# A gated linear attention and two MLPs on one core: the first step of the recurrence loaded and ordered another way, and v issued by another queue

## The chip, the cores and the metric

One core of one Trainium2 chip runs the whole program. The metric is the device time of that core in microseconds. The kernel before takes 954.99 us, the median of three runs (954.11 to 955.01). The execution that the profile shows took 954.32 us, and its span, from the first to the last recorded instruction, is 952.2 us.

## What is computed

```python
f = 1.0 / (1.0 + np.exp(-f_logit))            # q, k, v, f: 4 batches, 8 heads, 768 tokens, 48 columns
for t in range(S):
    state = f[:, :, t, :, None] * state + np.einsum('bhd,bhe->bhde', k[:, :, t], v[:, :, t])
    y[:, :, t] = np.einsum('bhd,bhde->bhe', q[:, :, t], state)
x = y.transpose(0, 2, 1, 3).reshape(B * S, H * D)      # 3072 tokens, 384 columns
x = (sigmoid(x @ w_gate) * (x @ w_val)) @ w_out        # 384 -> 1536 -> 384
h = x @ w_in                                           # 384 -> 2048
out = (h * sigmoid(1.702 * h)) @ w_out2                # 2048 -> 384
```

## The kernel before

The recurrence is cut into 12 steps of 64 tokens. A step has four units, one for each pair of heads (UG = 4), and a unit holds the four batches side by side: 256 columns (W) on 2 x 48 partitions. Units are numbered through, so units 0 to 3 are the first step, 4 to 7 the second. For a unit ScalarE makes the gates (`forget`), VectorE makes two products of gates by scans (`begin_decay`, `end_decay`), GpSimd multiplies k and q by them (`decay_k`, `decay_q`), and TensorE works in visits. A visit turns k of one unit (`k_turned`, copied by `take_k`), makes its scores, which VectorE masks, and in the same visit or the next one makes the y and the new state of a unit whose scores are masked. ScalarE copies y out of PSUM (`take_y`), for later steps VectorE adds the part within the step (`add_y`), and DMAs of SyncE move y to its rows of x (`move_y`, two or three DMAs a unit, as the 48 rows of a head cross a slab of 128).

The MLPs run over groups of tokens: two groups of 256 (steps 0 and 1), then groups of 512. A group of the first MLP has twelve blocks of 128 hidden columns. Every product is made of three matmuls in the fp32r format (w_hi by x_hi, w_hi by x_lo, w_lo by x_hi), so a block is 9 matmuls for the gate, 9 for the value and 9 for the output of the block before. x and the weights are split for it into hi (ScalarE casts) and lo (VectorE subtracts): `x_first_part` and `x_second_part`, `w1_first_part` and `w1_second_part`. The weights of the first MLP come in twelve pieces of 1152 columns that pass through three slots in `stage` and one in `final`; they are loaded and split ahead of their blocks in group 0.

Before the first block TensorE makes eight visits, which bring step 0's y into x. Later visits lie between the value and the output of blocks named in `VISIT_AT`: five in group 0 (they make the y of step 1), eight in group 1 (the y of steps 2 and 3, which group 2 reads), eight in each later group. `FORGET_AT` and `PREPARE_AT` say in which block the gates and the decays of a unit are made. Each engine runs its list in order. In block q ScalarE makes the sigmoid, waits for VectorE's product, casts `act_hi`, and then does what else is due (`take_k`, `forget`, `take_end`, `take_y`, a piece of w1, at block 10 `x_first_part` of the next group). TensorE may start the gate of block q only when the sigmoid of block q - 1 is done (`sig_done`), and its value when VectorE's product of block q - 1 is done (`mul_done`). Where x of a new group is split, ScalarE waits in its list for every y that has to be there (`y_moved`), and its next sigmoid stands behind that.

SyncE's list in a block with a visit is `load_f` of a coming unit, `load_kq`, `load_v`, `move_y` of the unit just made, in an order that depends on the block. All are DMAs of SyncE's one queue; each costs that queue its issue time. ScalarE's queue issues w1 from piece 1 on and, for the first step, f and v. At the start SyncE loads k and q of units 0 to 3 one unit after another, w1 piece 0, then moves y; ScalarE loads f and v unit by unit in between its work. TensorE's `keep_warm(n)` makes n products that nobody reads. Before the first block TensorE waits for all moves of y.

## Time and profile before

| | |
|---|---|
| median of 3 runs | 954.99 us |
| the profiled execution | 954.32 us |
| its span | 952.2 us |
| TensorE busy | 931.2 us, 98% |
| VectorE, ScalarE, GpSimd busy | 45%, 35%, 11% |
| first matmul of the first MLP | 28.57 us |

The page gives the totals; the timelines give what happened when. In a timeline an instruction has its start, its duration, its line of the kernel, what it writes and reads, and in brackets how long its engine had been idle before it and who ended that. SPq and ACTq are DMA issues in the lists of SyncE and ScalarE. A matmul's duration overlaps its neighbour's, so the pace of TensorE is read from the distance of two starts. The granted clock of TensorE is 1.00 at 2.4 GHz and 0.50 at 1.2 GHz.

### The profile page before, as it was taken

Reading aid. Unit: us, or ns where it says so; the run is one execution under the profiler, and the core shown is the slowest. Engines: PE = TensorE matmul, PEld = TensorE weight load, DVE = VectorE, ACT = ScalarE, POOL = GpSimd, SP = SyncE. Lnnn points to the kernel's source line nnn. Section 1 sums busy time; section 2 is a strip of 40 time slices with the busy share of each in tenths; the row PEclk is TensorE's granted clock in tenths of the full one; section 3 lists DMA queues with packets and bytes.
Section 4 is the critical chain, followed back from the end, with each engine's and each line's share of the span. In section 5 each row is a group of like instructions: output and inputs, shape, how many; then the busy total and the mean of one; then the engine's idle time right before and its main releaser. Section 6 shows DMA issues by size and latency. Waiting matters only on the chain.

```text
span 952.2 us, 17778 instructions
## 1 busy us (share of the span) xinstructions
PE 931.2 (98%) x7147; PEld 779.8 (82%) x7147; DVE 433.1 (45%) x789; ACT 335.9 (35%) x753; POOL 107.0 (11%) x126
## 2 busy tenths in 40 slices
PE   7899979999999999999999999999999999999997
PEld 5899968888888888888888888888888888888886
DVE  5697645437445544644333234343443443443433
ACT  3564433334333333333324333332232332232332
POOL 4112211102111111211004420000000000000000
PEclk6899989999999999999999999999999999999999
DMA  5863322222321321130223330010010200200000
GB/s 142 220 164 70 78 66 62 57 48 51 73 50 40 78 64 43 34 88 15 63 67 100 100 84 0 1 67 1 16 52 0 67 1 1 67 0 1 34 1 35
DMA packets 108374, 52.34 MB, mean 55 GB/s; under 512 B 95488, under 2 KB 100096, under 8 KB 108288
## 3 DMA queue, kind: packets, MB, share of 16 engines
q1 hardware_dynamic: 103312, 43.67, 18.2%
q10 hardware_dynamic: 4976, 7.49, 2.6%
q8 instruction: 58, 0.95, 0.4%
q14 instruction: 28, 0.23, 0.1%
HBM read 36.96 MB, written 9.44 MB: 49 GB/s over the span
## 4 chain that ended last, share of the span: by engine, by line
PE 92%; SPq 2%; DMA 2%; ACTq 1%; ACT 1%; DVE 1%; issue 1%; DVEq 0%
PE up_ps L1080 17%; PE up_ps L1082 17%; PE up_ps L1081 17%; PE out_ps L1080 13%; PE out_ps L1081 12%; PE out_ps L1082 12%; DMA f_raw<-f_t 2%; PE att_ps L1046 2%; PE att_ps L1064 1%; PE att_ps L1073 1%; PE att_ps L1055 1%; PE turn_ps L1025 1%; SPq L413 1%; SPq L406 1%; SPq L382 1%
## 5 line engine op out<-in xcount | busy, mean ns | idle before, releaser
L1080 PE MATMUL up_ps<-x_hi,w_hi 128*128 128x512 f32 (+1 forms) x792 | 294.9, 372 | 9.5 <-ACT act_f L710 9.5
L1082 PE MATMUL up_ps<-x_hi,w_lo 128*128 128x512 f32 (+1 forms) x792 | 294.4, 372 | 0.0
L1081 PE MATMUL up_ps<-x_lo,w_hi 128*128 128x512 f32 (+1 forms) x792 | 294.3, 372 | 0.0
L1080 PE MATMUL out_ps<-act_hi,w_hi 128*128 128x512 f32 (+1 forms) x540 | 207.8, 385 | 0.7 <-DVE act_lo L941 0.7
L1081 PE MATMUL out_ps<-act_lo,w_hi 128*128 128x512 f32 (+1 forms) x540 | 203.0, 376 | 0.0
L1082 PE MATMUL out_ps<-act_hi,w_lo 128*128 128x512 f32 (+1 forms) x540 | 202.6, 375 | 0.0
L716 ACT CAST act_hi<-act_f 128x512 fp32r<-128x512 f32 (+1 forms) x180 | 106.6, 592 | 234.4 <-DVE act_f L927 162.1
L1080 PEld LDWEIGHTS up_ps<-x_hi,w_hi 128*128 128x128 f32 x792 | 150.4, 190 | 35.3 <-ACT act_f L710 7.0
L1082 PEld LDWEIGHTS up_ps<-x_hi,w_lo 128*128 128x128 f32 x792 | 150.3, 190 | 25.6
L1081 PEld LDWEIGHTS up_ps<-x_lo,w_hi 128*128 128x128 f32 x792 | 150.4, 190 | 25.5
L941 DVE TENSOR_TENSOR act_lo<-act_f,act_hi 128x512 fp32r<-128x512 f32 (+1 forms) x180 | 117.7, 654 | 78.7 <-ACT act_hi L716 78.7
L927 DVE TENSOR_TENSOR act_f<-act_f,up_ps 128x512 f32<-128x512 f32 (+1 forms) x84 | 51.2, 610 | 210.9 <-PE up_ps L1082 205.1
L930 DVE TENSOR_TENSOR act_f<-act_f,up_ps 128x512 f32<-128x512 f32 x96 | 66.0, 687 | 173.4 <-ACT act_f L712 173.4
L712 ACT ACTIVATE act_f<-up_ps 128x512 f32<-128x512 f32 x96 | 57.4, 598 | 193.0 <-PE up_ps L1082 193.0
L1080 PEld LDWEIGHTS out_ps<-act_hi,w_hi 128*128 128x128 f32 x540 | 101.8, 189 | 22.0 <-DVE act_lo L941 1.2
L1082 PEld LDWEIGHTS out_ps<-act_hi,w_lo 128*128 128x128 f32 x540 | 101.9, 189 | 18.6
L1081 PEld LDWEIGHTS out_ps<-act_lo,w_hi 128*128 128x128 f32 x540 | 101.9, 189 | 17.1
L710 ACT ACTIVATE act_f<-up_ps 128x512 f32<-128x512 f32 (+1 forms) x84 | 45.0, 536 | 128.9 <-PE up_ps L1082 128.5
L543 POOL TENSOR_TENSOR k_dec<-k_raw,after_prod 128x256 f32<-128x256 f32 x48 | 41.7, 868 | 313.0 <-DVE after_prod L801 240.6
L642 ACT COPY y_t<-att_ps 48x128 f32<-48x128 f32 x176 | 45.7, 260 | 16.2 <-DVE state L839 14.7
L811 DVE TENSOR_TENSOR_SCAN to_prod<-gate,starts 128x264 f32<-128x264 f32 x44 | 40.2, 913 | 0.0
L533 POOL TENSOR_TENSOR q_dec<-q_raw,to_prod 128x256 f32<-128x256 f32 x48 | 33.0, 687 | 54.8 <-issue 42.9
(74 smaller groups left out, 516.5 us busy)
## 6 DMA issues: line engine op xcount, KB each, us to landing
stage<-w SPq DMA_DIRECT2D x16, 384.0 KB, 3.3
k_raw<-k_t SPq DMA_DIRECT2D x96, 48.0 KB, 2.1
q_raw<-q_t SPq DMA_DIRECT2D x96, 48.0 KB, 2.1
stage<-w ACTq DMA_DIRECT2D x8, 576.0 KB, 4.4
x_dram<-final SPq DMA_DIRECT2D x36, 128.0 KB, 2.4
x_raw<-x_dram SPq DMA_DIRECT2D x6, 768.0 KB, 4.7
out_t<-final SPq DMA_DIRECT2D x18, 256.0 KB, 2.3
v_raw<-v_n SPq DMA_DIRECT2D x88, 48.0 KB, 2.3
```

Source lines behind the costliest of these rows:

```text
L543: pool.tensor_tensor(by_chunk(k_dec[:, u.s, :]), by_chunk(k_raw[:, u.s, :]), chunks(after_prod, u.s)[:, :, 2:], ALU.mult).then_inc(k_dec_d ...
L642: last = act.copy(y[rows[i], :, r, :], banks(v)[rows[r], i, STATE_COL:STATE_COL + BLOCKS * C].rearrange("p (c t) -> p c t", c=BLOCKS))
L710: act.activation(act_f[:, b.t, 0:b.n], up_ps[:, 0, 0:b.n], ACT.Sigmoid).then_inc(sig_done, 1)
L712: act.activation(act_f[:, b.t, 0:b.n], up_ps[:, b.j % 2, 0:b.n], ACT.Sigmoid, scale=1.702).then_inc(sig_done, 1)
L716: act.copy(act_hi[:, b.t, 0:b.n], act_f[:, b.t, 0:b.n]).then_inc(act_hi_done, 1)
L811: dve.tensor_tensor_scan(to_prod[:, u.s, :], gate_of(n), starts[:, u.s, :], 1.0, ALU.mult, ALU.max).then_inc(scan_done, 1)
L927: dve.tensor_tensor(act_f[:, b.t, 0:b.n], act_f[:, b.t, 0:b.n], up_ps[:, 1, 0:b.n], ALU.mult).then_inc(mul_done, 1)
L930: dve.tensor_tensor(act_f[:, b.t, 0:b.n], act_f[:, b.t, 0:b.n], up_ps[:, b.j % 2, 0:b.n], ALU.mult).then_inc(mul_done, 1)
L941: dve.tensor_tensor(act_lo[:, b.t, 0:b.n], act_f[:, b.t, 0:b.n], act_hi[:, b.t, 0:b.n].bitcast(F32), ALU.subtract).then_inc(act_split, 1)
L1080: pe.matmul(dst, w_hi[:, at:at + P], m_hi, start=first, stop=False)
L1081: pe.matmul(dst, w_hi[:, at:at + P], m_lo, start=False, stop=False)
L1082: return pe.matmul(dst, w_lo[:, at:at + P], m_hi, start=False, stop=last)
```

## The change

- The first step's f, k and q come in one pair of DMAs each for all four units (f of unit 0 also by itself, ahead), and v in four DMAs, all issued by SyncE. They land in space that is free so early: f in `act_f`, k in the slot of w1 piece 2, q in the slot of piece 3. So piece 2 is loaded by SyncE after the four `decay_k` and three `move_y`, and piece 3 by ScalarE after the four `decay_q`. The slots of later units are cleared by GpSimd instead.
- The visits of the first step are split into parts and ordered anew: scores of units 0 and 1, y of 0, scores of 2, y of 1, scores of 3, y of 2 and 3; only then the states of 0 to 3, with the turns of k of units 2 and 3. There are twelve visits instead of eight, with the same products in sum. They use more PSUM banks, and the two decay products of units 2 and 3 have places of their own.
- Of each unit's y the first head (rows 0 to 47) is copied from PSUM straight into x, by ScalarE for units 0 and 1 and by VectorE for 2 and 3 (`put_y`); the second head is moved by DMA as before, so there are five moves in step 0 instead of ten.
- The states of step 0 are copied by ScalarE (`take_state`), the casts of the first three pieces of w1 are made by GpSimd, and `take_end` goes from ScalarE to GpSimd for all units.
- Unit 4's gates are still made ahead of the first block, but its decays are now made in block 0 of group 0, its visit lies in block 1 instead of 0, and the other visits of group 0 in blocks 3, 4, 6, 8 instead of 2, 4, 6, 8.
- From group 1 on `load_v` is issued by ScalarE, right after `take_y`, instead of by SyncE ahead of `move_y`.
- TensorE makes five unread products behind each of the first four `after_done`, and other numbers of them later.

```diff
-    VISITS = []
-    for n in range(UG):
-        VISITS += [(n, None), (None, n)]
+
+    VISITS = [(0, 0, None, None), (1, 1, None, None), (None, None, None, 0), (None, 2, None, None), (None, None, None, 1),
+              (None, 3, None, None), (None, None, None, 2), (None, None, None, 3),
+              (None, None, 0, None), (2, None, 1, None), (3, None, 2, None), (None, None, 3, None)]
     BEFORE_MLP = len(VISITS)
...
+    VISITS += [(UG, UG, None, None)] + [(n, n, n - 1, n - 1) for n in range(UG + 1, UNITS)] + [(None, None, UNITS - 1, UNITS - 1)]
...
-        for j in (0, 2, 4, 6, 8) if g == 0 else (0, 1, 3, 4, 5, 7, 8, 9):
+        for j in (1, 3, 4, 6, 8) if g == 0 else (0, 1, 3, 4, 5, 7, 8, 9):
...
-            FORGET_AT.update({(g, j): n + 6 for n, j in enumerate((0, 2, 4, 6, 8, 10))})
-            PREPARE_AT.update({(g, j): n + 5 for n, j in enumerate((0, 2, 4, 6, 8, 10))})
+            FORGET_AT.update({(g, j): n + 5 for n, j in enumerate((0, 1, 3, 5, 7, 9, 11))})
+            PREPARE_AT.update({(g, j): n + 4 for n, j in enumerate((0, 1, 2, 4, 6, 8, 10))})
...
+                sp.wait_ge(gaps_set, 1)
+                for i in range(PAIR):
+                    sp.dma_start(by_batch(f_raw[rows[i], 0, :]), f_steps[0, i, :, :, 0:C]).then_inc(f_loaded[0], 16)
+                sp.wait_ge(gaps_set, 2)
+                for i in range(PAIR):
+                    sp.dma_start(all_units(f_first[rows[i], :]), f_units[i, :, :, 0:C]).then_inc(first_f_loaded, 16)
                 sp.wait_ge(gaps_set, 3)
-                load_k(0)
+                for i in range(PAIR):
+                    sp.dma_start(all_units(k_first[rows[i], :]), k_units[i, :, :, 0:C]).then_inc(first_k_loaded, 16)
                 sp.wait_ge(q_gaps_set, 1)
-                load_q(0)
-                for n in range(1, UG):
-                    load_kq(n)
+                for i in range(PAIR):
+                    sp.dma_start(all_units(q_first[rows[i], :]), q_units[i, :, :, 0:C]).then_inc(first_q_loaded, 16)
+                for r in range(SIDES):
+                    for c in range(BLOCKS):
+                        sp.dma_start(v_raw[halves[r], 0:UG, c, :], v_units[r, c, 0:C, :, 0, :]).then_inc(first_v_loaded, 16)
                 sp.dma_start(w1_staged(0), w1[:, 0:PIECE1]).then_inc(w1_loaded[0], 16)
+                load_f(4)
+                load_kq(4)
                 move_y(0)
-                load_k(4)
                 move_y(1)
-                load_q(4)
-                move_y(2, slice(2, 3))
-                move_y(3, slice(1, 2))
-                load_v(4)
+                move_y(2)
+
+                sp.wait_ge(k_dec_done, UG)
+                sp.dma_start(w1_staged(2), w1[:, 2 * PIECE1:3 * PIECE1]).then_inc(w1_loaded[2], 16)
                 load_f(5)
                 load_kq(5)
+                load_v(4)
                 load_f(6)
+                load_kq(6)
                 load_v(5)
-                load_kq(6)
                 load_f(7)
                 load_v(6)
                 load_v(7)
...
@@ -471,7 +551,8 @@
                         if early:
                             load_kq(turned + 3)
                         if made is not None:
-                            load_v(made + 4)
+                            if b.g == 0:
+                                load_v(made + 4)
                             move_y(made)
...
-                pool.memset(q_raw[:, :, :], 0.0).then_inc(q_gaps_set, 1)
                 pool.memset(x_raw[:, 0, :], 0.0).then_inc(warm_set, 1)
+                pool.memset(starts[:, :, :], SAFE_PRODUCT).then_inc(starts_set, 1)
+                pool.wait_ge(starts_set, 1)
+                pool.memset(starts[:, :, :].rearrange("p s (c t) -> p s c t", c=CH)[:, :, :, C + 1], 1.0).then_inc(starts_set, 1)
+                pool.memset(q_first, 0.0).then_inc(q_gaps_set, 1)
                 pool.memset(ident[:, :], 0.0).then_inc(steps_set, 1)
                 pool.memset(causal[:, :], 1.0).then_inc(steps_set, 1)
                 pool.wait_ge(steps_set, 2)
...
-                pool.memset(gate[:, :, :], 0.0).then_inc(gate_gaps_set, 1)
+                pool.memset(f_raw[:, 1, :], 30.0).then_inc(slot_gaps_set, 1)
+                pool.memset(k_raw[:, :, :], 0.0).then_inc(slot_gaps_set, 1)
+                pool.memset(q_raw[:, :, :], 0.0).then_inc(slot_gaps_set, 1)
+                pool.memset(y_t[:, :, :], 0.0).then_inc(slot_gaps_set, 1)
 
...
+                def w1_first_part(t):
+
+                    pool.wait_ge(w1_loaded[t], 16)
+                    pool.tensor_copy(w_hi[:, t * PIECE1:(t + 1) * PIECE1], w1_staged(t)).then_inc(first_w1_hi_done, 1)
+
+                for n in range(3):
+                    decay_k(n)
+                decay_q(0)
+                decay_q(1)
+                decay_k(3)
+                decay_q(2)
+                decay_q(3)
+                for n in range(UG):
+                    take_end(n)
+
+                pool.wait_ge(p_end_done, UG)
+                pool.memset(gate[:, :, :], 0.0).then_inc(gate_gaps_set, 1)
+                for t in range(AHEAD):
+                    w1_first_part(t)
 
                 for g in range(NG1 - 1):
                     for j in range(J1):
...
+                def load_v(n):
+                    if n < UNITS:
+                        u = Unit(n)
+                        act.wait_ge(visit_done, out_visit[n - 4] + 1)
+                        for r in range(SIDES):
+                            act.dma_start(v_raw[halves[r], n % 4, :, :], v_chunks(u, r)).then_inc(v_loaded[n % 4], 16)
...
+                def put_y(n):
+
+                    v = out_visit[n]
+                    act.wait_ge(visit_done, v + 1)
+                    for src, slab, dst in pieces_put(n):
+                        act.copy(x_raw[dst, slab, 0:W].rearrange("p (c r t) -> p c r t", c=BLOCKS, r=SIDES),
+                                 banks(v)[src, :, Y_COL:STATE_COL].rearrange("p r (c t) -> p c r t", c=BLOCKS)).then_inc(y_put_by_act, 1)
+
+                def take_state(n):
+
+                    v = keep_visit[n]
+                    act.wait_ge(visit_done, v + 1)
+                    if n == 0:
+
+                        act.wait_ge(q_dec_done, UG)
+                    act.copy(by_side(state[:, n, :, :]), products_of(v)).then_inc(first_state_done, 1)
...
-                first_load_f(0)
 
                 act.wait_ge(warm_set, 1)
-                act.activation(y_t[:, 0, 0:1], x_raw[:, 0, 0:1], ACT.Sigmoid)
-                act.wait_ge(gaps_set, 2)
-                first_load_f(1)
+                act.activation(k_rows[:, 0, 0, 0:1], x_raw[:, 0, 0:1], ACT.Sigmoid)
                 forget(0)
-                first_load_f(2)
-                first_load_v(0)
                 forget(1)
-                first_load_f(3)
-                first_load_v(1)
+                forget(2)
+                forget(3)
                 take_k(0)
-                forget(2)
-                first_load_v(2)
-                take_end(0)
-                forget(3)
-                first_load_v(3)
                 take_k(1)
                 take_y(0)
-                take_end(1)
+                put_y(0)
+                take_y(1)
+                put_y(1)
                 load_w1(1)
-                first_load_f(4)
+                take_y(2)
+                take_y(3)
+                first_move_y(3)
                 take_k(2)
-                take_y(1)
-                take_end(2)
+                take_state(0)
+                take_k(3)
+                x_first_part(0)
+                take_state(1)
+                take_state(2)
+                take_state(3)
                 forget(4)
-                take_k(3)
-                take_y(2)
-                first_move_y(2, slice(0, 2))
-                take_end(3)
-                w1_first_part(0)
-                take_y(3)
-                first_move_y(3, slice(0, 1))
-                load_w1(2)
-                take_end(4)
-                x_first_part(0)
-                w1_first_part(1)
                 load_w1(3)
-                forget(5)
-                w1_first_part(2)
                 load_w1(4)
 
                 for q, b in enumerate(BLOCK):
...
             def _(dve):
 
                 dve.memset(f_raw[:, 0, :], 30.0).then_inc(gaps_set, 1)
-                dve.memset(f_raw[:, 1, :], 30.0).then_inc(gaps_set, 1)
-                dve.memset(k_raw[:, :, :], 0.0).then_inc(gaps_set, 1)
-
-                for at in (0, C + 1):
-                    dve.memset(up_ps[:, :, 0:SPACED].rearrange("p s (c t) -> p s c t", c=CH)[:, :, :, at], 0.0).then_inc(gaps_set, 1)
-                for ps in (att_ps, out_ps):
...
 
-                dve.wait_ge(gaps_set, 7)
                 dve.wait_ge(starts_set, 2)
-                begin_decay(0)
-                end_decay(0)
-                begin_decay(1)
-                after_visit(0)
-                end_decay(1)
-                begin_decay(2)
-                after_visit(1)
-                after_visit(2)
-                end_decay(2)
+                for n in range(3):
+                    begin_decay(n)
+                    end_decay(n)
                 begin_decay(3)
-                after_visit(3)
-                after_visit(4)
                 end_decay(3)
-                after_visit(5)
-                after_visit(6)
-                begin_decay(4)
-                after_visit(7)
-                end_decay(4)
-                decay_state(4)
+                after_visit(score_visit[0])
+                after_visit(score_visit[1])
+                after_visit(score_visit[2])
+                after_visit(score_visit[3])
+                put_y(2)
+                put_y(3)
                 w1_second_part(0)
                 x_second_part(0)
                 w1_second_part(1)
...
+                    pe.matmul(turn_ps[:, 0:384], x_raw[:, 0, 0:P], x_raw[:, 0, 0:384], start=True, stop=True)
                 pe.wait_ge(consts_set, CONSTS)
+                for n in range(UG):
+                    pe.wait_ge(after_done, n + 1)
+                    keep_warm(5, turn_ps)
+
...
-                                                     v_raw[halves[r], made % 4, c, cols[i]], start=False,
+                                    last = pe.matmul(ps[halves[i], r, at], k_rows[halves[r], kept % 2, c, halves[i]],
+                                                     v_raw[halves[r], kept % 4, c, cols[i]], start=opens and c == 0,
                                                      stop=False, skip_group_check=True)
-                    if turned is not None:
-                        pe.wait_ge(q_dec_done, turned + 1)
+                        opens = False
...
                             for i in range(PAIR):
-                                last = pe.matmul(ps[rows[c % SIDES], i, at], state[rows[i], m.p, c, :],
+                                last = pe.matmul(ps[rows[c % SIDES], i, at], state[rows[i], made % UG, c, :],
                                                  q_dec[rows[i], made % 4, c * C:(c + 1) * C], start=False, stop=False,
                                                  skip_group_check=True)
                     last.then_inc(visit_done, 1)
+                    if turned is not None and v < UG:
+                        turn()
 
                 def products(dst, at, m_hi, m_lo, first, last):
...
                 for v in range(BEFORE_MLP):
+                    if v == 3:
+
+                        pe.wait_ge(scan_done, UG)
                     visit(v)
-                    keep_warm(1)
-
-                wait_y(pe, 3)
-                keep_warm(3)
+                    keep_warm({0: 0, 1: 0, 3: 1, 5: 1, 7: 2}.get(v, 0))
+
                 for slot in (0, 1, 2):
                     pe.wait_ge(y_moved[slot], 16 * moves(slot, UG))
                     keep_warm(3)
 
-                pe.wait_ge(scan_done, UG)
-                pe.wait_ge(state_done, UG)
+                pe.wait_ge(first_state_done, 2)
 
                 for b in BLOCK:
```

## Rows read from the trace of the kernel before

**Rows 1.** TensorE's waits, whole run: engine, line, releaser: us, times, longest.
```profile
PE up_ps L1080 <- ACT act_f L710: 9.5, 3, 5.8
```

**Rows 2.** Timeline of TensorE: start us, us, instruction, [idle before it].
```profile
28.57 0.40 PE L1080 MATMUL up_ps<-x_hi,w_hi 128*128 128x256 f32 x1
...
34.47 0.35 PE L1080 MATMUL up_ps<-x_hi,w_hi 128*128 128x256 f32 x1 [2.86 <-ACT act_f L710]
...
108.61 0.39 PE L1080 MATMUL up_ps<-x_hi,w_hi 128*128 128x256 f32 x1 [0.88 <-ACT act_f L710]
...
129.34 0.28 PE L1081 MATMUL out_ps<-act_lo,w_hi 128*128 128x256 f32 x1
129.46 0.28 PE L1082 MATMUL out_ps<-act_hi,w_lo 128*128 128x256 f32 x1
135.49 0.80 PE L1080 MATMUL up_ps<-x_hi,w_hi 128*128 128x512 f32 x1 [5.75 <-ACT act_f L710]
```

**Rows 3.** Stretches: us, busy PE, PEld, DVE, ACT, POOL, clock, DMA share, GB/s.
```profile
8.00:28.50 20.50, 17.84 (x220) 14.90 (x220) 11.84 (x25) 7.43 (x21) 5.40 (x8) 0.50 0.62 171
35.40:38.90 3.50, 3.50 (x19) 3.50 (x18) 3.47 (x6) 1.83 (x5) 1.37 (x2) 0.51 0.91 265
40.00:60.00 20.00, 20.00 (x330) 19.26 (x329) 18.46 (x35) 13.44 (x34) 3.46 (x5) 1.00 0.73 203
85.80:133.00 47.20, 42.85 (x680) 40.91 (x675) 28.47 (x66) 20.07 (x67) 9.13 (x12) 1.00 0.34 79
135.50:141.20 5.70, 5.70 (x13) 4.45 (x14) 3.17 (x7) 1.41 (x4) 1.62 (x2) 0.50 0.22 47
```

**Rows 4.** Timeline of ScalarE: the instructions behind TensorE's three stalls.
```profile
32.59 0.42 ACT L602 ACTIVATE gate<-f_raw 128x256 f32<-128x256 f32 x1 [5.30 <-DMA f_raw<-f_t]
...
106.77 0.42 ACT L602 ACTIVATE gate<-f_raw 128x256 f32<-128x256 f32 x1 [3.59 <-DMA f_raw<-f_t]
...
134.53 0.62 ACT L657 CAST x_hi<-x_raw 128x512 fp32r<-128x512 f32 x1 [3.22 <-DMA x_raw<-y_t]
```

**Rows 5.** Timelines of SyncE's queue and VectorE at the end of group 1.
```profile
91.62 1.37 SPq L406 DMA_DIRECT2D v_raw<-v_n  x2
...
124.01 0.42 DVE L849 TENSOR_TENSOR y_t<-y_t,att_ps 128x256 f32<-128x256 f32 x1 [0.94 <-ACT y_t L642]
...
131.86 1.21 SPq L413 DMA_DIRECT2D x_raw<-y_t  x2
```

**Rows 6.** SyncE's queue, 85.8 to 133 us, waited for: us, times, longest.
```profile
SPq L413 <- DVE y_t L849: 0.4, 1, 0.4
```

**Rows 7.** Timeline of ScalarE: idle before a block's sigmoid, groups 1 and 2.
```profile
100.90 0.38 ACT L710 ACTIVATE act_f<-up_ps 128x256 f32<-128x256 f32 x1 [0.40 <-PE up_ps L1082]
...
212.83 0.60 ACT L710 ACTIVATE act_f<-up_ps 128x512 f32<-128x512 f32 x1 [2.35 <-PE up_ps L1082]
```

**Rows 8.** ScalarE's own issues of v in the first step: ns min/median/max.
```profile
L619 ACTq DMA_DIRECT2D v_raw<-v_n x8: 602/626/749, 5.2 to 11.5; - x8
```

**Rows 9.** Timelines of VectorE, GpSimd and TensorE in the first step.
```profile
5.40 0.71 DVE L811 TENSOR_TENSOR_SCAN to_prod<-up_ps,starts 128x264 f32<-128x264 f32 x1
...
6.25 0.68 POOL L533 TENSOR_TENSOR q_dec<-q_raw,to_prod 128x256 f32<-128x256 f32 x1 [0.27 <-DVE to_prod L811]
...
15.02 0.71 PE L1064 MATMUL att_ps<-q_dec,k_dec 48*64 48x64 f32 x16
...
23.43 5.42 PE L1010 MATMUL out_ps<-ident 128*128 128x128 f32 x24 [1.55 <-ACT y_t L638]
```

**Rows 10.** Timeline of VectorE: w_lo without and with GpSimd work beside it.
```profile
27.32 1.36 DVE L871 TENSOR_TENSOR w_lo<-stage,w_hi 128x1152 fp32r<-128x1152 f32 x1 [0.60 <-ACT w_hi L583]
...
37.29 1.85 DVE L871 TENSOR_TENSOR w_lo<-stage,w_hi 128x1152 fp32r<-128x1152 f32 x1
```

**Rows 11.** GpSimd by line and shape: count, busy us, mean ns.
```profile
L555 POOL TENSOR_TENSOR w_lo<-stage,w_hi 128x768 fp32r<-128x768 f32 x16 | 29.3, 1841 | 83.4 <-ACT w_hi L590 83.4
```

**Rows 12.** Loads of w1 into stage, 0 to 60 us.
```profile
DMA to landing us min/median/max: 4.0/4.4/6.4
```

293 lines of the change are left out of this document (184 added, 109 removed).

## The prediction

> **What bounds the kernel now.** I read the page's totals first, and they say little by themselves: TensorE is busy in 98% of the span, so a change can only win what is in the other 2% and what ran at half the clock. So the next view is who TensorE waited for. One line stands out: the first matmul of a block's gate waited three times for ScalarE's sigmoid, 9.5 us in all [rows 1]. The timeline shows where: 2.86 us at 34.47, 0.88 us at 108.61 and 5.75 us at 135.49 [rows 2]. Third, the table by stretches, for the clock. It was 0.50, the lower level of 1.2 GHz, from 8 us to the first block, and again for 3.5 us behind the first stall and for 5.7 us behind the third [rows 3]. At half the clock a stretch does half its work, so the two cost 1.75 and 2.85 us more. The three stalls and the two slow stretches are 2.86 + 1.75 + 0.88 + 5.75 + 2.85 = 14.1 us. The rest of the loss is the time before the first block, 28.57 us [rows 2].
>
> Each sigmoid was late because ScalarE stood in its list at something older. At 32.59 and 106.77 it waited for the f of a unit (5.30 and 3.59 us), at 134.53 for a moved y, 3.22 us for the last slab [rows 4]. Who was late there? Between 85.8 and 133 us SyncE's queue waited for data only 0.4 us on a y and not much more in all [rows 6]; it was issuing, while the DMA engines were busy 0.34 of the time [rows 3]. VectorE had finished the last y of group 1 at 124.01 + 0.42 = 124.43, and its move was issued at 131.86, 7.4 us later [rows 5]. So the bound at the end of group 1 is the issue time of one queue, not bandwidth and not arithmetic.
>
> **v to ScalarE.** In that stretch SyncE issues seven pairs for v like the one of 1.37 us [rows 5]; they take 1.35 to 1.86 us each, some 10 us. Without them the queue is 10 us shorter where it was 7.4 us late, so it catches up and then waits for each y. The last move would start right behind 124.43 and take 1.21 us; before, the cast that waited for it began 1.46 us after its issue had ended (134.53 against 131.86 + 1.21) [rows 4, 5], which puts it at 127.1. The cast (0.62 us) and the sigmoid behind it end by 128.4. TensorE wants the next gate at 129.46 + 0.12 = 129.6 [rows 2]. The stall of 5.75 us goes with 1.2 us to spare, and with it the half clock behind it, 2.85 us. The f at 106.77 was issued late for the same reason, behind two to three of the seven pairs, and with it goes 0.88 us. Sum: 9.5 us.
>
> The cost is on ScalarE: two issues of 0.63 us [rows 8], 1.25 us a visit, less a `take_end`. It was idle 0.40 us before a sigmoid in group 1 and 2.35 us in a group of 512 [rows 7]. In group 1 the sigmoid comes 0.85 us later. It lasts 0.38 us, and TensorE has at least 18 matmuls of 0.12 us (value and output [rows 2]) before it needs it, 2.16 us. So it is hidden; in larger groups the idle time alone covers it. I take 0. If the cover were gone, it would be 1.25 us in each of 36 visits. The added wait, for the visit itself, is one that `take_y` has already passed.
>
> Beside [rows 3, 5], the Trainium skill says (Perfetto Trace Analysis, DMA Optimizations) that when the issuing of DMAs is the bottleneck, spreading it over other engines may help; the trace agrees with its condition, a solid queue and a share of 0.34. Its page DMA: Bandwidth & Descriptors (Issuing engines are not separate DMA queues) speaks against the gain: another issuing engine saves only the issue time, "which is usually small relative to the DMA itself". By that the term would be near 0 and the sum 952.1; it is the first rival.
>
> **The start.** Now k, q and f of four units come in single pairs. I put 0.39 MB for each of the three at the 171 GB/s of the old start [rows 3]: 2.3 us each, so f, k and q land near 5.8, 8.1 and 10.4 us. VectorE's eight scans of 0.71 us [rows 9] and the small instructions between them take 1.66 us a unit: from 4.45, one scan ahead of the one at 5.40, to 11.1 or 12 us. GpSimd's products of 0.68 us [rows 9] wait for k and q and give the first scores at about 11 us, and TensorE is through its unread products at about 12.1. Then it has 16 bundles, four each of scores, y, states and turns, at about 0.6 us apart at half clock (one lasts 0.71 with overlap [rows 9]): 9.6 us. Thirteen `keep_warm` products follow or lie between at 5.42 / 12 = 0.45 us each [rows 9]: 5.9 us. First block at 12.1 + 15.5 = 27.6, a gain of 1.0 us. The engine copies and the halved moves take work off the old chain (y copied, moved, landed), but they lie beside TensorE's own list, which is now the later one; I count them at nothing. Bounds: at full clock TensorE's list shrinks to 8 us and the chain through the copies and moves is last, first block near 23 (gain 5.5); with q landing late and a late piece of w1, near 30.5 (loss 2). I take the end near half clock, because small matmuls did not raise the clock in all of the old start [rows 3].
>
> **Group 0.** The stall of 2.86 us goes: f of unit 4 is loaded early, and f of unit 5 is no longer behind three `load_v` and moves. What is late next is VectorE. It was busy 18.46 of 20 us in this group [rows 3] with decays in every second block. Now unit 4's decays move behind the first product, so blocks 0, 1 and 2 in a row each hold two scans and a `w_lo` of 1.36 us [rows 10] beside the four usual instructions: some 4.2 us, an estimate from these rows, against 27 x 0.12 = 3.24 us for TensorE. The lag is 2.9 us by block 3; part of it is absorbed by the spare time at the first block and by visit 12. I take a stall of 1.7 us; bounds 0 and 2.9. Piece 3 of w1 is now issued after unit 4's gates, some 2 us before the first block, and lands 4.0 to 6.4 us after its issue [rows 12]; ScalarE casts it in block 0 and the sigmoid of block 1 stands behind. It just fits; it costs up to 2 us where it doesn't, in the same place as VectorE's lag, not on top. The clock has been at half before the first block, with fewer unread products just ahead of it (nine, where there were twelve), so I add 1.0 us of slow first blocks; bounds 0 and 1.75. Old loss 4.6, new loss 2.7: gain 1.9 us.
>
> The casts of three pieces go to GpSimd. A cast of 1152 columns is not in the trace; its subtraction with two inputs took 1.84 us for 768 [rows 11], so at most 2.8 us each. They are needed one block after another and the third is ready by the start of block 1. I take 0 on the path. Against it stands a row: `w_lo` took 1.85 us instead of 1.36 with GpSimd at work beside it [rows 10]. Three of those are 1.5 us, in the upper bound. By the Trainium skill (SBUF — State Buffer, Who interferes with whom) a VectorE instruction with two inputs in SBUF contends with GpSimd's reads; the trace agrees with its 0.49 us, and with all three on the path the sum would be 944.1.
>
> **The sum.** 9.5 + 1.0 + 1.9 = 12.4 us off the profiled execution of 954.32 us (span 952.2, and 2.1 around it) is 941.9. The median lies 0.7 above that execution: 942.6.
>
> **Rivals.** *First, the moves stay late.* The seven pairs leave SyncE, but the issues that stay get longer when ScalarE issues at the same time, or SyncE comes to wait in its list. For: issues are uneven already (1.35 to 1.86 us for the same pair). Against: 10 us are taken from a queue that is 7.4 late. With half the gain of group 1: 947.4; with none: 952.1. *Second, the clock stays high in the start*, thanks to twenty unread products behind the scans. For: they are of the kind that stood before the first block when the clock rose [rows 3, 9]. Against: twenty of them lie before the visits, and the small matmuls of the visits did not hold the clock up. First block near 23 and no slow blocks: 942.6 - 4.5 - 1.0 = 937.1. *Third, the start slips.* Four large loads share the DMA engines, nothing can be scored before all of q is there, and TensorE's list has four more visits. First block near 31 instead of 27.6: 946.0; this price is certain to reach the end, as nothing hides a later first block. *Fourth, slower: v in ScalarE's list.* The mechanism is the sigmoid standing behind two issues in 36 visits. It decides from 12.4 / 36 = 0.34 us a visit that reaches TensorE; at 0.5 us it is 942.6 + 18 = 960.6. Against it is the idle time of 0.40 and 2.35 us [rows 7]; for it only that an issue could wait for the other queue's. That the change doesn't do what it says, v staying on SyncE's path by another wait, is the first rival with no gain.
>
> **Chances and range.** Forecast, 940 to 945.5: 0.55. First rival 0.17, second 0.14, third 0.08, fourth 0.06. The range of 937.0 to 949.5 takes in the forecast, half of the first rival, most of the second and the third. A measurement of this kernel can tell about 0.2%, 1.9 us, from no change. Faster by more than that 0.91, within 0.03, slower 0.06.
>
> **What would show it.** Right: no idle time of TensorE near the first block of group 2 and the clock at 1.00 there; SyncE's queue waiting for VectorE's y in group 1; seven or eight pairs for v in ScalarE's list with its sigmoids unhurried; the first gate matmul at 27 to 28 us; a wait of 1 to 2 us in blocks 2 or 3 of group 0 that ends with VectorE's `w_lo`. Wrong: a stall at group 2 left; a first block before 25 or after 30; waits for ScalarE's sigmoid spread over later groups. The term I trust least is the start, as it hangs on the clock; the one that would break the sum is the 9.5 us.

## The result, and the profile after

| | before | after |
|---|---|---|
| median, six runs each | 955.00 us | 938.16 us (937.35 to 938.94) |
| ratio | | 0.9825, 95% interval 0.9812 to 0.9837 |
| the profiled execution | 954.32 us | 937.35 us, span 935.6 |
| first matmul of the first MLP | 28.57 us | 22.28 us |

The gain is 16.8 us; the forecast was 12.4. The view of who TensorE waited for, in the changed kernel (engine, line, releaser: us, times, longest), is short. It answers [rows 1], where one line held 9.5 us. Its first five lines are:

```profile
PE turn_ps L1128 <- DVE after_prod L921: 1.5, 2, 1.0
PE turn_ps L1132 <- POOL x_raw L590: 1.4, 1, 1.4
PE att_ps L1204 <- POOL q_dec L621: 1.0, 1, 1.0
PE up_ps L1222 <- ACT act_f L829: 1.0, 1, 1.0
PE up_ps L1222 <- DVE w_lo L998: 0.9, 1, 0.9
```

Of the four lines left out, one is 0.8 us near the end of the program, as before (0.7), and the others are 0.3 us each. The first two lines shown are before the first visit. The other three are all in group 0 or at its end, as TensorE's timeline of the changed kernel shows (it answers [rows 2]); at 122.04 is the first gate of group 2, which had waited 5.75 us:

```profile
22.28 0.36 PE L1222 MATMUL up_ps<-x_hi,w_hi 128*128 128x256 f32 x1
...
28.43 0.46 PE L1204 MATMUL att_ps<-q_dec,k_dec 48*64 48x64 f32 x16 [1.03 <-POOL q_dec L621]
...
34.26 0.38 PE L1222 MATMUL up_ps<-x_hi,w_hi 128*128 128x256 f32 x1 [0.86 <-DVE w_lo L998]
...
71.17 0.38 PE L1222 MATMUL up_ps<-x_hi,w_hi 128*128 128x256 f32 x1 [0.99 <-ACT act_f L829]
...
122.04 0.47 PE L1222 MATMUL up_ps<-x_hi,w_hi 128*128 128x512 f32 x1
```

The table by stretches of the changed kernel (us, busy PE, PEld, DVE, ACT, POOL, clock, DMA share, GB/s), to be laid beside [rows 3]:

```profile
8.00:22.20 14.20, 13.36 (x255) 11.13 (x256) 9.90 (x20) 6.23 (x19) 8.50 (x15) 1.00 0.98 218
28.00:32.00 4.00, 3.56 (x42) 3.53 (x43) 3.97 (x7) 2.13 (x5) 1.31 (x3) 1.00 0.91 235
36.00:40.00 4.00, 4.00 (x89) 3.75 (x88) 4.00 (x7) 1.11 (x5) 1.47 (x3) 1.00 0.72 213
80.00:118.50 38.50, 38.50 (x646) 37.01 (x645) 23.70 (x60) 17.43 (x57) 9.13 (x15) 1.00 0.43 97
122.00:128.00 6.00, 6.00 (x88) 4.96 (x88) 5.37 (x12) 2.11 (x5) 2.23 (x4) 1.00 0.28 62
```

Two things are new: the clock is 1.00 from 8 to 22 us, where it was 0.50, and VectorE has no idle time from 28 to 40 us.

To see where the gain came in, read the same sigmoid in both kernels: the first of group 1 and the third of group 2. Of before (two rows not shown so far), then of after:

```profile
78.83 0.38 ACT L710 ACTIVATE act_f<-up_ps 128x256 f32<-128x256 f32 x1
...
147.20 0.60 ACT L710 ACTIVATE act_f<-up_ps 128x512 f32<-128x512 f32 x1 [1.21 <-PE up_ps L1082]
```
```profile
72.55 0.38 ACT L829 ACTIVATE act_f<-up_ps 128x256 f32<-128x256 f32 x1 [0.16 <-PE up_ps L1224]
...
131.04 0.60 ACT L829 ACTIVATE act_f<-up_ps 128x512 f32<-128x512 f32 x1 [1.20 <-PE up_ps L1224]
```

| stretch | gain at its end | gain in it | forecast |
|---|---|---|---|
| to the first block | 28.57 - 22.28 = 6.29 | 6.3 | 1.0 |
| group 0 | 78.83 - 72.55 = 6.28 | 0.0 | 1.9 |
| group 1 and the first blocks of group 2 | 147.20 - 131.04 = 16.16 | 9.9 | 9.5 |
| the rest | 954.32 - 937.35 = 16.97 | 0.8 | 0 |

### The profile page after: what moved, and what is told of

The parts are those of the page before. It is cut to its first block, busy times and chain, and to the rows that moved or that the text cites. A ratio compares the mean times of both kernels' runs of the same rounds, so it can differ in the third digit from the quotient of the medians.

```text
span 935.6 us, 17906 instructions
## 1 busy us (share of the span) xinstructions
PE 923.4 (99%) x7173; PEld 773.0 (83%) x7173; DVE 434.8 (46%) x789; ACT 328.8 (35%) x709; POOL 137.1 (15%) x181
## 4 chain that ended last, share of the span: by engine, by line
PE 95%; DVE 2%; issue 1%; DMA 1%; SPq 0%; ACT 0%; ACTq 0%; DVEq 0%
PE up_ps L1222 17%; PE up_ps L1224 17%; PE up_ps L1223 17%; PE out_ps L1222 13%; PE out_ps L1223 12%; PE out_ps L1224 12%; PE att_ps L1182 2%; PE att_ps L1204 1%; PE turn_ps L1152 1%; PE att_ps L1193 1%; PE att_ps L1213 1%; DMA act_f<-f_t 0%; PE out_ps L1128 0%; DVE w_lo L998 0%; DVE after_prod L921 0%
## 5 line engine op out<-in xcount | busy, mean ns | idle before, releaser
L635 POOL TENSOR_TENSOR k_dec<-k_raw,after_prod 128x256 f32<-128x256 f32 x44 | 39.4, 895 | 284.4 <-issue 281.2
L653 POOL TENSOR_TENSOR w_lo<-stage,w_hi 128x768 fp32r<-128x768 f32 x16 | 29.3, 1842 | 83.4 <-ACT w_hi L705 83.4
```

The costliest lines, as they stand in the source:

```text
L635: pool.tensor_tensor(by_chunk(k_dec[:, n % 4, :]), k, chunks(after_of(n))[:, :, 2:], ALU.mult).then_inc(k_dec_done, 1)
```

## The experiments

Lines with + and - are against the kernel named. Each ratio is to the kernel before, run beside it on the same chip.

### v alone, undone and done

*Undone:* the changed kernel with v issued by SyncE everywhere.

```diff
-                            if b.g == 0:
-                                load_v(made + 4)
+                            load_v(made + 4)
                             move_y(made)
...
-                        if b.g:
-                            load_v(made + 4)
```

> The changed kernel with v issued by SyncE again in all groups, ahead of the move of y. Theory (the end of group 1 is bound by the issue time of SyncE's queue): seven pairs of 1.35 to 1.86 us come back into that queue, the last move of y is again issued some 7 us after VectorE's last sum, TensorE stalls 4 to 6 us ahead of the first block of group 2 and then runs about 5 us at half clock. 938.2 + 9.5 = 947.7 us, between 945.5 and 949. Rival (the gain of group 1 comes from the new start, which leaves the queue less behind): within 1 us of 938.2. A rival in between (the new start gives the queue a lead, so only part comes back): 941 to 944.

Measured: 947.93 us (945.39 to 950.80), ratio 0.9931 [0.9907, 0.9956]; 9.8 us more than with the change. The stall at group 2 is back with its clock; TensorE's waits and the stretch behind it:

```profile
PE up_ps L1219 <- ACT act_f L828: 6.8, 2, 6.0
...
131.00:136.00 5.00, 5.00 (x17) 3.87 (x16) 1.62 (x3) 0.60 (x1) 2.04 (x3) 0.65 0.26 59
```

*Done alone:* the kernel before with v issued by ScalarE from group 1 on, nothing else.

```diff
-                            load_v(made + 4)
+                            if b.g == 0:
+                                load_v(made + 4)
                             move_y(made)
...
                         take_y(made)
+                        if b.g:
+                            load_v(made + 4)
```

> The kernel before with only this part of the change: v issued by ScalarE from group 1 on. Theory (queue issue time): the stalls of 0.88 and 5.75 us and the 5.7 us at half clock go, 955.0 - 9.5 = 945.5 us, between 944 and 947.5; the stall of 2.86 us in group 0 and the first block at 28.6 us stay. Rival (v in ScalarE's list delays its sigmoids): 950 or more, with TensorE's waits for the sigmoid spread over the later groups. If the parts add up, this gain and what e1 gives back agree within 1.5 us.

Measured: 946.01 us (945.70 to 946.39), ratio 0.9910 [0.9881, 0.9938]: 8.9 us below the 954.87 of the kernel before beside it. Of the three waits for the sigmoid only the one in group 0 is left, and ScalarE casts x for group 2 without waiting:

```profile
PE up_ps L1090 <- ACT act_f L718: 2.6, 1, 2.6
...
126.62 1.66 ACT L665 CAST x_hi<-x_raw 128x512 fp32r<-128x512 f32 x3
```

So the term is 9 to 10 us by three ways: 9.8 undone, 8.9 alone, 9.9 in the timelines. The first rival with no gain is out. The forecast quoted the Trainium skill (DMA: Bandwidth & Descriptors, Issuing engines are not separate DMA queues): another issuing engine saves only the issue time, which is usually small relative to the DMA itself. The runs agree with both halves: what left SyncE's queue was issue time, and a DMA of v costs 0.7 us to issue (1.35 a pair) and takes 2.3 us from issue to landing, in the median. What failed is the rival's step from there to a gain near 0. Fourteen such issues in a queue that is never idle are 10 us, and TensorE waited for what stood behind them.

### How much room the queue has

The changed kernel, from group 1 on, with one of the two v DMAs of a unit on SyncE and one on ScalarE.

```diff
-                            if b.g == 0:
-                                load_v(made + 4)
+                            load_v(made + 4, range(SIDES) if b.g == 0 else (0,))
...
-                        for r in range(SIDES):
+                        for r in (1,):
                             act.dma_start(v_raw[halves[r], n % 4, :, :], ...)
```

> The changed kernel with one of the two DMAs of each v from group 1 on issued by SyncE and the other by ScalarE. Theory (issue time of the queue against a fixed lateness): about 5 of the 10 us come back into a queue that had 3 to 5 us to spare, so the last move is at most 1 to 3 us late; a stall of 0 to 2 us at group 2 and no half clock: 938.2 to 940.5 us. Rival (each issue on SyncE costs TensorE its share, in proportion): half of 9.5 us, 943 us. Rival (two queues that issue at once lengthen each other's issues): SyncE's issues longer than in the changed kernel, and 941 or more.

Measured: 942.18 us (941.61 to 942.58), ratio 0.9871 [0.9843, 0.9899]. That is above the first theory (938.2 to 940.5) and 0.8 us under the second (943). The third gave 941 or more, but its condition did not come: the 56 other DMAs of the queue took 33.7 us to issue here and 35.1 in the changed kernel, so they got no longer. Seven issues, 5.5 us in sum, went back. The last y was done at 116.39, and its move was issued at 120.90, 4.5 us later. TensorE stood 2.81 us at 124.50, the longest of two waits, and the clock was 0.69 behind it, where the first theory expected no half clock:

```profile
PE up_ps L1221 <- ACT act_f L828: 3.1, 2, 2.8
...
120.90 1.18 SPq L482 DMA_DIRECT2D x_raw<-y_t  x2
...
123.55 0.62 ACT L791 CAST x_hi<-x_raw 128x512 fp32r<-128x512 f32 x1 [3.35 <-DMA x_raw<-y_t]
...
124.50:130.00 5.50, 5.50 (x17) 4.39 (x18) 3.18 (x7) 1.33 (x3) 2.17 (x3) 0.69 0.29 64
```

So of the 5.5 us only about 1 us found room. The changed kernel's own rows show the same. SyncE's queue and VectorE's last y of group 1:

```profile
110.58 1.97 SPq L456 DMA_DIRECT2D k_raw<-k_t  x2
112.59 0.93 SPq L463 DMA_DIRECT2D q_raw<-q_t  x2
113.62 1.79 SPq L482 DMA_DIRECT2D x_raw<-y_t  x3
115.45 1.26 SPq L449 DMA_DIRECT2D f_raw<-f_t  x2
116.81 1.20 SPq L482 DMA_DIRECT2D x_raw<-y_t  x2
...
116.32 0.42 DVE L973 TENSOR_TENSOR y_t<-y_t,att_ps 128x256 f32<-128x256 f32 x1 [0.94 <-ACT y_t L758]
```

In this execution the queue issues without a gap at the end of the group; it is free at 116.71, the y is there at 116.74, and its move starts at 116.81. It has caught up, with nothing to spare. Other executions with v on ScalarE's queue have more. Over group 1 the queue waited for VectorE's y once in the changed kernel, near the group's start, and for 7.4 us where v alone was moved:

```profile
SPq L482 <- DVE y_t L973: 2.9, 1, 2.9
...
SPq L413 <- DVE y_t L859: 7.4, 2, 6.5
```

### v in the later groups

The changed kernel with v issued by ScalarE in group 1 alone, and by SyncE again from group 2 on.

```diff
-                            if b.g == 0:
+                            if b.g != 1:
                                 load_v(made + 4)
...
-                        if b.g:
+                        if b.g == 1:
                             load_v(made + 4)
```

> The changed kernel with v issued by ScalarE in group 1 alone and by SyncE again from group 2 on. If the gain of moving v comes from group 1 and ScalarE's list has room in the later groups (it was idle 2.35 us before a sigmoid there), nothing changes: 937.9 to 938.5 us, and no wait of TensorE's near the starts of the later groups. If the two issues a visit cost TensorE something in the later groups, which is the fourth rival in small, it is faster: by 0.1 us a visit, 28 visits, 935.4 us. If SyncE is late in the later groups too, it is slower and shows a wait for ScalarE's sigmoid at the start of group 3 or later.

Measured: 937.53 us (936.89 to 938.14), ratio 0.9825 [0.9807, 0.9843]: no difference, and no stall at a later group. The move pays in group 1 alone, and in 28 later visits costs nothing that can be told. Group 1 is the same program as in the changed kernel, yet here SyncE's queue waited 2.5 us for VectorE's y between 80 and 118 us, where it waited for none in the changed kernel's profile. The last move was issued 0.03 us after its y. So how much room the queue has differs from execution to execution.

### The clock in the start

The changed kernel without the twenty unread products behind the scans.

```diff
-                for n in range(UG):
-                    pe.wait_ge(after_done, n + 1)
-                    keep_warm(5, turn_ps)
```

> The changed kernel without the twenty unread products that TensorE makes behind the first four scans; nothing that is computed changes. Theory (they keep TensorE's clock at its upper level through the visits of the first step): the granted clock falls to 0.50 from about 8 or 12 us until the first block or beyond, the visits and the unread products behind them stretch, the first block starts at 25 to 27.5 us instead of 22.5 and its first 3 us may run at half clock: 941.5 to 944.5 us. Rival (the visits of the new order hold the clock up by themselves, or the first block waits for the moves of y and w_lo, not for TensorE): within 0.8 us of 938.2, the first block before 23.3.

Measured: 943.23 us (942.63 to 944.35), ratio 0.9884 [0.9856, 0.9913]. TensorE waits 7.52 us for the first unit's q, up to 12.64. The granted clock is 0.50 from 8 us, in that wait, to the first block, which comes at 28.36; the visits run at half pace:

```profile
12.00:16.00 4.00, 3.36 (x68) 2.50 (x68) 1.21 (x3) 0.85 (x3) 3.94 (x10) 0.50 0.85 217
...
24.50 4.12 PE L1128 MATMUL out_ps<-ident 128*128 128x128 f32 x18
28.36 0.38 PE L1219 MATMUL up_ps<-x_hi,w_hi 128*128 128x256 f32 x1
```

In the changed kernel the same eighteen matmuls took 2.27 us at 20.25. Is the clock alone the gain, then? The kernel before with eight unread products more at the start and three instead of one behind each visit:

```diff
+                keep_warm(8)
...
                     visit(v)
-                    keep_warm(1)
+                    keep_warm(3)
```

> The kernel before with more unread products in its first step: eight at the start and three instead of one behind each of its eight visits; nothing that is computed changes. Theory (the clock is what the new start gains most by, and density of full-size products holds it): the granted clock stays above 0.50 in part or all of the 8 to 28.5 us, the visits come closer together, and the first block starts 1 to 4 us earlier: 951 to 954 us. Rival (the old start is bound by its loads, moves and copies, and TensorE's own pace there costs nothing): the first block at 28 to 30 us and 954 to 957 us, whatever the clock does. It can't be read if the clock stays at 0.50 with them.

Measured: 955.73 us (953.71 to 956.74), ratio 1.0005 [0.9991, 1.0019]: nothing gained, though the clock was 1.00 to 20 us. TensorE got to the last unit's y sooner (18.29 us, where it was 20.08) and then stood idle for copies of ScalarE:

```profile
4.00:20.00 16.00, 14.66 (x246) 11.87 (x244) 8.43 (x19) 3.23 (x12) 5.43 (x9) 1.00 0.76 190
20.00:24.00 4.00, 1.31 (x22) 1.07 (x22) 2.34 (x6) 2.27 (x6) 1.36 (x2) 0.86 0.10 26
...
20.96 0.45 PE L1056 MATMUL out_ps<-v_raw,k_rows 64*64 64x48 f32 x16 [2.22 <-ACT k_rows L624]
...
24.26 5.49 PE L1010 MATMUL out_ps<-ident 128*128 128x128 f32 x24 [1.99 <-ACT y_t L638]
29.39 0.51 PE L1081 MATMUL up_ps<-x_hi,w_hi 128*128 128x256 f32 x1
```

The four together, as time of the first gate matmul:

| | half clock in the visits | full clock in the visits |
|---|---|---|
| old order and loads | 28.57 us | 29.39 us |
| new order and loads | 28.36 us | 22.28 us |

Neither gained anything alone in these runs; together they are worth 6.3 us. At half clock TensorE's own list is the last thing in the new order, and all but a wait of 1.55 us [rows 9] in the old one; with the visits at full clock the old order is held up by ScalarE's copies, 2.22 and 1.99 us. The run of the old order is no clean cell of the table, though. It makes 24 unread products more, and its clock fell in the second of those waits, so that the last 24 matmuls took 5.49 us. By the pace of the eighteen in 2.27 they would take about 3 (an estimate), and the first gate matmul would stand near 26.9. The old order at full clock to its end was not run.

Then the changed kernel with eight unread products instead of twenty:

```diff
-                    keep_warm(5, turn_ps)
+                    keep_warm(2, turn_ps)
```

> The changed kernel with two unread products behind each pair of scans of the first step instead of five: eight instead of twenty. With twenty the clock was 1.00 in the whole start, the first gate matmul stood at 22.28 us and the median was 938.16; with none the clock was 0.50 from 8 to 28 us, the first gate matmul stood at 28.36 and the median was 943.23. Theory A, it is the sum of work between the scans that counts, so that eight are too little: clock 0.50 through most of the visits, first gate matmul at 26.5 to 28.5, 942 to 943.5 us. Theory B, any product between the scans is enough: clock 1.00, first gate matmul at 22.1 to 22.6, 938 us. I hold A for likelier, at 2 to 1; a clock that falls only late in the visits, with a first gate at 23.5 to 26 and 939.5 to 941.5 us, would stand between them.

Measured: 943.54 us (942.95 to 944.39), ratio 0.9874 [0.9858, 0.9889]; as with none. The first gate matmul is at 27.90. Here the record of the clock misleads. It says 1.00, yet the scores take 0.71 us, as at half clock [rows 9], where they took 0.46 with twenty:

```profile
5.39 1.06 PE L1128 MATMUL turn_ps<-ident 128*128 128x128 f32 x4
8.12 1.22 PE L1128 MATMUL turn_ps<-ident 128*128 128x128 f32 x4 [1.67 <-DVE after_prod L921]
...
12.39 0.71 PE L1204 MATMUL att_ps<-q_dec,k_dec 48*64 48x64 f32 x16
...
12.00:16.00 4.00, 4.00 (x72) 2.76 (x70) 0.99 (x3) 1.10 (x3) 3.94 (x10) 1.00 0.69 189
```

Four such matmuls take 1.22 us here, as in the kernel without any (at 19.70), and 0.71 in the changed kernel (at 16.95). The four at 5.39, ahead of the wait, were slow too: 1.06 us for four, where the changed kernel made ten in 1.35:

```profile
5.72 1.35 PE L1128 MATMUL turn_ps<-ident 128*128 128x128 f32 x10 [0.54 <-DVE after_prod L921]
```

So by the pace this execution was at half clock from 5.39 us at the latest, and it cannot show where a clock that has risen is lost. What the times show is that eight are too few: all four executions took 942.95 to 944.39 us. Where the clock is lost is shown by the kernel without any (the wait of 7.52 us) and by the kernel before with more of them (the wait of 1.99).

### What holds the start at full clock

The changed kernel with every y of the first step moved by DMAs and none put into x by engines.

```diff
-            return [piece for piece in pieces_of_pair(n % UG) if n >= UG or piece[0].start >= 64]
+            return pieces_of_pair(n % UG)
...
+                        act.copy(y[rows[0], :, :, :], banks(v)[rows[0], :, Y_COL:STATE_COL]...)
...
-                put_y(0)
...
-                put_y(1)
...
-                put_y(2)
-                put_y(3)
```

> The changed kernel with all of the first step's y moved into x by DMA (ten moves instead of five), its first head copied to y_t by ScalarE instead of into x; no copies by VectorE. Theory of the prediction (the copies lie beside TensorE's own list and are worth nothing) held for half clock; at full clock the chain through the moves is last: SyncE issues seven of them, 0.6 us each, three to four more than now, so the cast of x begins some 2 to 3 us later and the first block with it: 940 to 941.5 us. Rival (TensorE's unread products or w_lo set the first block also at full clock): within 0.8 us of 938.2.

Measured: 940.55 us (939.99 to 942.06), ratio 0.9862 [0.9845, 0.9879]; 2.4 us worse, the first gate at 23.88. The copies and issues stand in ScalarE's list, and TensorE waits for a `take_k` behind them. That is another path than the one expected, the moves; ScalarE's cast of x did wait 0.72 us for one. TensorE's wait:

```profile
PE turn_ps L1148 <- ACT k_rows L741: 1.7, 2, 1.5
```

Next, the changed kernel with one unread product instead of three behind each wait for moved y, six fewer, 1.5 us:

```diff
                     pe.wait_ge(y_moved[slot], 16 * moves(slot, UG))
-                    keep_warm(3)
+                    keep_warm(1)
```

> The changed kernel with one instead of three unread products behind each of the three waits for moved y: six fewer, 1.5 us of TensorE's time just ahead of the first gate matmul (the eighteen recorded at 20.25 took 2.27 us). x_hi is ready at 21.26 and the first x_lo about 0.45 us behind its start at 20.46, so the first gate matmul could start at 21.3 instead of 22.28. Theory A, the end is set by the first block: 938.16 - 1.0 = 937.2 us. Theory B, VectorE, which was busy 3.97 to 4.00 of every 4 us from 28 to 40 us, sets the pace of group 0's first blocks, so an earlier first block only waits longer: 937.9 to 938.4. Theory C, the clock falls with fewer unread products: above 939, with a granted clock or a pace of half in 20 to 32 us. I hold B for likelier.

Measured: 936.87 us (936.44 to 938.75), ratio 0.9823 [0.9803, 0.9842]: too close to tell from the changed kernel by the times. The rows say more. The first gate is 0.46 us earlier, not 1.0, since ScalarE is now last, and the two waits in the first blocks keep their length (1.03 and 0.87), so that the profiled span is 0.6 us shorter:

```profile
21.82 0.38 PE L1222 MATMUL up_ps<-x_hi,w_hi 128*128 128x256 f32 x1 [0.60 <-ACT state L777]
...
33.81 0.39 PE L1222 MATMUL up_ps<-x_hi,w_hi 128*128 128x256 f32 x1 [0.87 <-DVE w_lo L998]
```

So theory B fell in this profile: the waits for VectorE move with the first block. Why is argued, not shown: VectorE's first product of group 0 waits 1.66 us for TensorE's value in the changed kernel, so its work there starts later or earlier with TensorE's.

### The new waits of group 0

At 71.17 TensorE waited 0.99 us. Followed back in the changed kernel, the sigmoid stood behind a cast of x that waited 2.98 us for a move, and SyncE had issued that move late, behind an f that stood in its list for the gates of another unit (the queue issued nothing from 63.04 to 64.40, and the gates end at 64.37):

```profile
63.96 0.41 ACT L724 ACTIVATE gate<-f_raw 128x256 f32<-128x256 f32 x1
...
64.40 1.88 SPq L449 DMA_DIRECT2D f_raw<-f_t  x2
...
67.77 1.21 SPq L482 DMA_DIRECT2D x_raw<-y_t  x2
...
70.43 0.40 ACT L792 CAST x_hi<-x_raw 128x256 fp32r<-128x256 f32 x1 [2.98 <-DMA x_raw<-y_t]
```

The changed kernel with that unit's gates one block earlier:

```diff
-... enumerate((0, 1, 3, 5, 7, 9, 11))})
+... enumerate((0, 1, 3, 5, 7, 8, 11))})
```

> The changed kernel with the gates of unit 10 made in block 8 of group 0 instead of block 9. In the changed kernel the load of f for unit 12 stands first in SyncE's list of block 8 and waits for these gates, with the last y of step 1 behind it; TensorE stalls 0.99 us at the first block of group 1. Theory (head of the queue): SyncE no longer waits there, the move is issued some 2 us earlier, the stall of 0.99 us goes: 937.2 us, between 936.6 and 937.9. Rival (the move is late through the pairs issued ahead of it, not through the wait): 938.2 within 0.5 us, the stall stays.

Measured: 937.66 us (937.18 to 938.00), ratio 0.9826 [0.9809, 0.9842], and the wait is 0.23 us:

```profile
70.73 0.38 PE L1222 MATMUL up_ps<-x_hi,w_hi 128*128 128x256 f32 x1 [0.23 <-ACT act_f L829]
```

The cause is shown by the row; the time moved by 0.5 us, within the intervals.

The changed kernel with unit 4's gates and decays ahead of the first block instead of in block 0:

```diff
                 take_k(3)
+                forget(4)
                 x_first_part(0)
...
-                forget(4)
...
                 w1_second_part(1)
+                begin_decay(4)
+                end_decay(4)
+                decay_state(4)
```

> The changed kernel with unit 4's decays made ahead of block 0 instead of in it (its gates ahead of the cast of x, its scans behind the second w_lo, its products on GpSimd behind the three casts). Theory (in blocks 0 to 2 VectorE has too much): TensorE's wait of 1.03 us for unit 4's q and its wait of 0.86 us for a w_lo go or shrink, and some of the 0.7 us of shorter gaps around them: 936.0 us, between 935.4 and 937.2. Rival (the work only moves onto the path ahead of the first block): the first block later by 0.3 to 1 us, the wait for w_lo unchanged at a later block, 937.5 to 939.

Measured: 937.97 us (937.65 to 938.80), ratio 0.9833 [0.9816, 0.9849]; the theory missed by 2 us, and the time is that of the rival. The wait of 1.03 us for `q_dec` went, and one of 1.12 took its place, as the scans now stand ahead of the product of block 0. The first block came 0.3 us later (22.57), and the wait for `w_lo` was 0.47 instead of 0.86:

```profile
27.17 0.39 PE L1226 MATMUL up_ps<-x_hi,w_hi 128*128 128x256 f32 x1 [1.12 <-DVE act_f L1049]
```

Both edits at once:

> Both small edits at once: the gates of unit 10 one block earlier (0.99 us of stall became 0.23, 937.66 us) and unit 4's decays ahead of the first block (937.97 us, where one wait of 1.03 went and one of 1.12 came). If the two only add, 938.16 - 0.50 - 0.19 = 937.5. Alone the second left a wait of 1.27 us at the first block of group 1, which is what the first one shortens, so their sum could be larger: 936.9 to 937.3. A result above 937.7 would say that the second gives nothing beside the first.

Measured: 937.45 us (936.36 to 937.55), ratio 0.9809 [0.9796, 0.9823]. They add and no more. Its interval overlaps that of the changed kernel, so that it is better is likely and not shown.

## Why the prediction was right or wrong

**The time** of 938.16 us lay in the range, near its lower end; the forecast of 942.6 was 4.4 us too high. The case that came is the second rival, at 0.14 and 937.1 us.

**"v to ScalarE", 9.5 us: right,** in mechanism and size (8.9, 9.8, 9.9). "It catches up and then waits for each y" is right in its first half and too strong in its second. The last move was issued 0.03 to 0.07 us after its y. But the queue waited for one to three of the y in group 1, not for each, and in the changed kernel's profile it issues without a gap near 116 us. That is why 5.5 us put back made TensorE stall for 2.81, though the forecast saw 10 us taken from a queue 7.4 us late. Two things used up its room. With TensorE's stall of 0.88 us gone the y come sooner: the last one was done 45.6 us behind the first gate matmul of group 1, where it was 46.9. And the DMAs that stay took longer in the changed kernel's profile, 35.1 us instead of 32.8. The first rival names a cause for that, ScalarE issuing at the same time, and the runs do not bear it out: the same 56 issues took 32.6 to 35.1 us in the runs with v on ScalarE's queue and 32.8, 33.4 and 35.1 in the three with all of v on SyncE's. The fourth rival asked for 0.34 us a visit; its price in the later groups is nothing that can be told, and in group 1 ScalarE is still idle 0.39 us before a sigmoid that follows a visit:

```profile
99.32 0.38 ACT L829 ACTIVATE act_f<-up_ps 128x256 f32<-128x256 f32 x1 [0.39 <-PE up_ps L1224]
```

**"The start", gain 1.0: the step that failed** is "I take the end near half clock, because small matmuls did not raise the clock in all of the old start". It took a clock that had been lost ahead of these matmuls for one that they can't hold. The rows of the kernel before show where it went. Its first unread products ran at full pace (0.49 us for two; at half it is 0.79), and the next bundle, behind a wait for v, at half:

```profile
7.38 0.49 PE L1010 MATMUL out_ps<-ident 128*128 128x128 f32 x2
8.79 0.68 PE L1046 MATMUL att_ps<-scores,v_raw 64*48 64x64 f32 x16 [0.92 <-DMA v_raw<-v_n]
```

With the pace held up to the first scores, the visits run at full pace from 12.45 to 20.25 us in the changed kernel. The kernel before with more unread products kept it through a wait of 2.22 us, too, and lost it in the next, of 1.99. What has to be asked is in which wait of TensorE's the clock is lost, and what it does ahead of that wait. The list that the step added up is good: at half clock it gave 27.6 for the first block and 15.5 us from the first scores, and the kernel without the unread products had 28.36 and 15.7, and 943.23 us against the forecast's 942.6. The bound for full clock, "near 23", was good too (22.28), but not for its reason: it had the chain of copies and moves last, and in the changed kernel TensorE's unread products end last, 0.5 us later than ScalarE's copies would let it start (the run with six fewer). The choice between the two clocks was the error, and it was worth 5.1 us.

**The engine copies "counted at nothing"** are worth 2.4 us at full clock. That they would be worth nothing at half clock is likely, as TensorE's list is then 6 us longer, but no run made it. So they should have stood in the second rival's sum.

**"Group 0", gain 1.9: mis-sized,** it was 0.0. The old loss of 4.6 us went. VectorE's lag came as described, without idle time in blocks 1 to 3, with `w_lo` at 1.85 to 1.87 us, and a wait of 0.86 us that ends with `w_lo` where 1.7 was taken. What the forecast missed is the other kind: 1.03 us at 28.43, where the scans of unit 4, now made in block 0, gave its q too late for the visit in block 1, and 0.99 us at 71.17, where SyncE stood at an f. The forecast had followed such a chain back for the old stalls, and did not follow the moved `forget` to who waits for it. The slow first blocks, 1.0 us, did not come, as the clock was up. These waits are 2.88 us, and yet the stretch gained nothing of the old 4.6. The distances of the blocks' first gate matmuls show the rest. At full pace a block takes 3.24 us, 4.71 with a visit of four bundles, some 4.0 with the first and smaller one (an estimate). In the changed kernel block 1 took 5.48 us (24.52 to 30.00), 1.5 too much; block 2 4.26, 1.0; blocks 3 to 5 4.80, 5.08 and 3.44, 0.7 in sum; block 11 4.39, 1.15. With some 0.1 us in block 0 that is 4.4 to 4.5 us, against 4.5 before. So a wait cost more than its idle time says, as the idle time counts only from the modelled end of the last matmul, and short ones around it are in no line.

**The casts on GpSimd** took 1.15 us each, not up to 2.8, and no wait of TensorE's for them shows. **The last 0.8 us** of the table are not explained; they are within what single executions differ by.

## What to carry to other kernels

Count a queue's issue time like an engine's busy time: with the DMA engines used for a third, seven pairs moved to another queue were worth 9 us, and only in the one group where the queue was last. Work out a start at both clocks and keep the two sums apart: the new order and loads gained 0.2 us here with the visits at half clock and 6.3 at full. When work is moved to an earlier or later block, follow each instruction that waits for it in the other engines' lists, the DMA queue's too.

## What the runs showed of the hardware

- A start can keep the full clock on small matmuls with few unread products between them: bundles of sixteen 48x64 matmuls ran in 0.44 to 0.46 us in the changed kernel and in 0.65 to 0.71 without the unread products behind the scans. With twenty of those the clock was up, with eight it was not; nothing between them was tried.
- The clock was lost in waits of different length: 0.92 us in the kernel before, 1.99 in the same kernel with more unread products, after a wait of 2.22 had not cost it.
- The granted clock of a stretch can read 1.00 while TensorE runs at half pace (0.71 us for sixteen score matmuls from 12.39 us, with eight unread products; that record reads 1.00 throughout). The pace of equal matmuls is the better witness.
- The price of issuing is uneven on a solid queue: the pair for k took 0.93 to 2.12 us. The 56 DMAs that stay on SyncE in group 1 took 35.1 us of issue time from 80 to 118.5 us in the changed kernel, and 42.8 - 10.0 = 32.8 from 85.8 to 133 before (summed over the timeline of the queue): 0.63 against 0.59 us for one. With v by SyncE again it was 0.60, with v moved alone 0.60, and over all runs it was 0.58 to 0.63 with v on ScalarE's queue and 0.59 to 0.63 with all of it on SyncE's. Whether ScalarE's issues lengthen them can't be told.
- A cast of 1152 columns to fp32r took GpSimd 1.15 us, where a subtraction of 768 with two inputs took 1.84 [rows 11].
